# A delta-rule attention with two expert layers: the queries' transposes, a down step and the split of the next weights put elsewhere

## The chip, the core and the metric

One NeuronCore of a Trainium2 chip runs the whole kernel in one launch. The metric is device microseconds from start to end of an execution; less is better. The engines are PE (TensorE, the matrix products), DVE (VectorE), ACT (ScalarE), POOL (GpSimd) and SP (SyncE, which here only issues transfers). Each has its own list of instructions, done in order, and waits for the others by semaphores.

## The reference

Three stages follow one another. Only what the change touches is shown in full.

```python
# 1: delta rule, batch 4, 8 heads, 768 tokens, head width 48
k_n = k / (norm(k) + 1e-06)
for t in range(S):
    y[:, :, t] = einsum('bhd,bhde->bhe', q[:, :, t], state)
    v_old = einsum('bhde,bhd->bhe', state, kt)
    state = state + bt * einsum('bhd,bhe->bhde', kt, vt - v_old)
# 2: four experts, N = 3072 tokens, D = 384, F = 1024
out += p[:, e:e + 1] * (maximum(x @ w1[e], 0.0) @ w2[e])
# 3: gated layer, F = 1536
(sigmoid(x @ w_gate) * (x @ w_val)) @ w_out
```

## The kernel before, in words

**Attention.** The 768 tokens are cut into 6 chunks of 128, and the 32 heads into two groups of 16. A window `w` (12 of them) is one chunk of one group. Within a window the recurrence becomes a triangular system of 128 by 128 per head. Its inverse is built by doubling: levels `l0` to `l4` work on blocks of 32 (line 790), each for two halves of 8 heads; a level's product goes from PE to DVE (mask, then a 32 by 32 transpose, lines 641 and 643) and to ACT (copy, line 561), and the next level needs both. The steps `m32y`, `m32z`, `m64y`, `m64z` then put blocks together.

The order of the work is written out by hand, in `slot(w, p, lev, rec, pre, moe)`. All engines run through the same list of calls, and each engine's own functions `lev`, `rec`, `pre`, `moe` say what it does at a call. A slot mixes four kinds of work: the levels of window `w`; the recurrence of window `w - 1` (`r(...)`: `u0` line 848, `au_a` and `au_b` lines 854 and 857, `u2` line 865, `y` lines 872 and 876, `s` line 884, whose sum into the state is DVE line 687); the preparation of window `w + 1` (`n(...)`); and a part of the first expert for window `w - 2` (`up` line 947, `down` line 956). In the first two slots, where there is no such window, PE does four stand-in products on constants (line 935) in the place of each up or down.

Preparation: `turn` transposes the unit keys on PE (line 892) and ACT copies them out; `product` is keys times keys (line 900), which DVE masks into `A` and `Ah` (lines 728 and 732); `first` (POOL line 528, DVE line 721) makes from `Ah` what level `l0` of the next slot needs. `turn_q` transposes the queries: 4 transposes for each half of the heads on PE, into `bank[0]` and `bank[1]`, and one ACT copy of 128x512 each into `KQ`. `product_q` is keys times queries (line 900 too), which DVE masks into `QK`, two operations of 128x512 for each half (line 739). `product_q` of half 1 writes the same two banks as half 0 and so waits until DVE has emptied them.

With window 1's second `turn_q`, DVE also normalizes the experts' weights (`early.normalize`, lines 999 to 1005).

**Experts.** The other half of expert 0 and the experts 1 to 3 run over 6 chunks of 512 tokens. For each block of 128 hidden units `f` PE does `up` (9 matmuls of 128x512), ACT makes the rounded high part (line 1130), DVE the low part (line 1165), and PE does `down` (12 matmuls of 128x384) one `f` later (lines 1194 to 1196). The weights of the next expert come by DMA as soon as the raw buffers are free and are split by ACT (`split1` line 1113 and `split2` line 1120) and by POOL (line 1100). Expert 0 has only 4 blocks `f` left, so ACT splits two blocks of each weight after each `f` there.

**Gated layer.** It is not touched.

The change lies in `slot`, in `run` and in the ACT block of `experts`, whose `split2` holds ACT until the raw weights have landed:

```python
def split2(e, f):
    if e:
        act.wait_ge(w2_in, 16 * e)
```

Of the kernel before, what the change touches and what calls it, by code (L numbers as in the profile page):

```python
# [60 lines left out]
def past(eng, semaphore, count):  # L61

    if not isinstance(count, int) or count > 0:
        eng.wait_ge(semaphore, count)


def delta_rule_attention(nc, q, k, v, beta, consts, places, x_hi, x_lo, ident, id_in, early, room, x_first, x_first_in):
# [9 lines left out]
    with ctx:  # L77
# [126 lines left out]
        def slot(w, p, lev, rec, pre, moe):  # L204

            m, has_next = w - 2, w < NW - 1

            def r(step, o):
                if w > 0 and not (step == "s" and w == NW - 1):
                    rec(step, w - 1, 1 - p, o)  # L210

            def n(step, which=None):
                if has_next:
                    pre(step, w + 1, 1 - p, which)

            def both(step):
                for hf in range(2):
                    lev(step, w, p, hf)

            def down(window, t, *fs):  # L220
                for f in fs:
                    moe("down", window, t, f)

            def up(f):
                for part in range(2):
                    moe("up", m, f, part)

            pre("value", w, p, None)
            both("l0")
            r("u0", 0)  # L230
            moe("weigh", m - 1, 0)
            n("square")
            down(m - 1, 1, 0, 1)
            both("l1")
            r("u0", 1)
            down(m - 1, 1, 2, 3)
            both("l2")
            moe("weigh", m - 1, 1)
            n("norm")
            n("unit", 0)  # L240
            n("unit", 1)
            r("au_a", 0)
            up(0)
            moe("low", m, 0)
            both("l3")
            r("au_b", 0)
            up(1)
            moe("low", m, 1)
            both("l4")
            both("blocks")  # L250
            both("quads")
            r("au_a", 1)
            n("turn", 0)
            rec("z", w, p, 0)
            both("m32y")
            r("au_b", 1)
            up(2)
            moe("low", m, 2)
            n("turn", 1)
            r("u2", 0)  # L260
            rec("z", w, p, 1)
            up(3)
            moe("low", m, 3)
            r("u2", 1)
            both("m32z")
            n("product", 0)
            r("y", 0)
            both("m64y")
            n("product", 1)
            down(m, 0, 0, 1)  # L270
            both("m64z")
            r("y", 1)
            pre("product_q", w, p, 0)
            r("s", 0)
            pre("product_q", w, p, 1)
            down(m, 0, 2, 3)
            r("s", 1)
            n("first", 0)
            n("first", 1)
            n("turn_q", 0)  # L280
            n("turn_q", 1)

        def run(lev, rec, pre, moe):
            for step, which in (("square", None), ("norm", None), ("unit", 0), ("unit", 1),
                                ("turn", 0), ("turn", 1), ("product", 0), ("product", 1),
                                ("first", 0), ("first", 1), ("turn_q", 0), ("turn_q", 1)):
                pre(step, 0, 0, which)
            for w in range(NW):
                slot(w, w % 2, lev, rec, pre, moe)
            m = NW - 2  # L290
            moe("weigh", m - 1, 0)
            for o in range(2):
                rec("u0", NW - 1, 1, o)
                for f in range(2 * o, 2 * o + 2):
                    moe("down", m - 1, 1, f)
            moe("weigh", m - 1, 1)
            for o in range(2):
                rec("au_a", NW - 1, 1, o)
                moe("up", m, o, 0)
                rec("au_b", NW - 1, 1, o)  # L300
                moe("up", m, o, 1)
                moe("low", m, o)
            rec("u2", NW - 1, 1, 0)
            moe("up", m, 2, 0)
            rec("u2", NW - 1, 1, 1)
            for o in range(2):
                rec("y", NW - 1, 1, o)
            moe("up", m, 2, 1)
            moe("low", m, 2)
            for part in range(2):  # L310
                moe("up", m, 3, part)
            moe("low", m, 3)
            for t in range(2):
                for f in range(KH):
                    moe("down", m, t, f)
                moe("weigh", m, t)
            for f in range(KH):
                for part in range(2):
                    moe("up", NW - 1, f, part)
                moe("low", NW - 1, f)  # L320
            for t in range(2):
                for f in range(KH):
                    moe("down", NW - 1, t, f)
                moe("weigh", NW - 1, t)
# [31 lines left out]
        with nc.Block() as block:  # L356
# [106 lines left out]
            def _(pool):  # L463
# [85 lines left out]
                def none(*_):  # L549
                    return  # L550

                run(lev, rec, pre, none)

            @block.scalar
            def _(act):
# [69 lines left out]
                def moe(step, m, f, part=1):  # L625
                    if step == "up" and part == 1 and m >= 0:
                        act.wait_ge(up_rdy, KH * m + f + 1)
                        past(act, dn_rdy, 2 * m)
                        nc.scalar.activation(hs[0][:, f, :], ebank[f % 2][:, 0:2 * P], ACT.Relu).then_inc(hh_done, 1)

                run(lev, rec, pre, moe)

            @block.vector
            def _(dve):
# [120 lines left out]

                nc.vector.memset(XTf[:, :, :].bitcast(F32), 0.0).then_inc(x_zeroed, 1)
                run(lev, rec, pre, moe)

            @block.tensor
# [250 lines left out]
def experts(nc, x_hi, x_lo, w1, w2, early, acc, w1raw, w2raw, w1_in, x_first, x_first_in, ahead):  # L1010
# [4 lines left out]
    E, D, F = w1.shape  # L1015
    N = x_hi.shape[1]
    KD, KF, NCK = D // P, F // P, N // T
    ctx = ExitStack()
    with ctx:
# [14 lines left out]
        def steps(g, e):  # L1034
            return KH * g if e == 0 else KF * g - (KF - KH) * NCK

        def todo(e):
            return KH if e == 0 else KF
# [17 lines left out]
        with nc.Block() as block:  # L1056
# [47 lines left out]
            @block.scalar  # L1104
            def _(act):
                def split1(e, f):

                    if e:
                        act.wait_ge(w1_in, 16 * e)
                    else:  # L1110
                        act.wait_ge(early.raw_in, 64)
                    raw, cols = w1raw if e else early.raw1, slice(P * f, P * (f + 1))
                    nc.scalar.activation(w1s[e % 2][0][:, :, cols], raw[:, :, cols], ACT.Copy).then_inc(w1_hi, 1)  # L1113
# [5 lines that stand above are left out]
                    raw = w2raw if e else early.raw2  # L1119
                    nc.scalar.activation(w2s[e % 2][0][:, f, :], raw[:, f, :], ACT.Copy).then_inc(w2_hi, 1)  # L1120

                def chunk(g, e, splits=None):
                    at = steps(g, e)
                    for f in range(todo(e)):
                        if isinstance(g, int) and g == 0 and f:
                            split2(0, f - 1)
                        i = f % NHB
                        act.wait_ge(h_rdy, at + f + 1)
                        past(act, o_used, at + f + 1 - NHB)
                        nc.scalar.activation(hs[i][0][:, :], bank[i][:, :], ACT.Relu).then_inc(hh_done, 1)  # L1130
                        if splits is not None:
                            per = KF // todo(e)
                            for n in range(per * f, per * (f + 1)):
                                split1(splits, n)
                                split2(splits, n)
                    if isinstance(g, int) and g == 0:
                        split2(0, KH - 1)

                for f in range(KH):
                    split1(0, f)  # L1140
                for e in range(E):
                    chunk(NCK * e, e)
                    chunk(NCK * e + 1, e, e + 1 if e + 1 < E else None)
                    with act.Fori(NCK * e + 2, NCK * (e + 1)) as g:
                        chunk(g, e)

            @block.vector
# [401 lines left out]
```

## Time and profile before

| | us |
|---|---|
| median of 3 runs | 1708.73 |
| lowest and highest | 1707.78, 1711.89 |
| profiled execution | 1704.52 |
| its span, first to last instruction | 1702.7 |
| PE busy | 1632.3 (96%) |
| DVE busy | 654.5 (38%) |
| ACT busy | 436.1 (26%) |
| POOL busy | 279.3 (16%) |

The attention with its part of expert 0 takes the first 520 us, the experts go to about 1235 us, the gated layer to the end. A slot of the attention takes about 38 us. PE is busy in nearly all of the span; what is left over is in short waits. The mean granted TensorE clock over the span is 0.987 of full speed: 1 is 2.4 GHz and 0.5 is 1.2 GHz, the only two levels in this trace.

### The profile page before, as it was taken

What the parts mean: (1) busy time and instruction counts of PE and PEld (TensorE: products, weight loads), DVE (VectorE), ACT (ScalarE), POOL (GpSimd) and SP (SyncE); (2) the same over time, 40 slices, a digit from 0 to 9 for tenths busy, and PEclk for the clock granted to TensorE, in tenths of its full rate; (3) what the DMA queues carried; (4) which work ended last, traced back from release to release, by engine and by line L of the source; (5) the groups of instructions that cost most, each with busy time, mean ns of one, the idle gap of its engine ahead of it and who ended that gap; (6) DMA issues with size and microseconds to landing.
All of it is one profiled execution on the core that took longest, in us unless ns stands there. A gap on an engine that the chain in (4) does not pass through costs nothing. (4 is left out here: it accounts for less than half of the span.)

```text
span 1702.7 us, 35068 instructions
## 1 busy us (share of the span) xinstructions
PE 1632.3 (96%) x14630; PEld 1462.4 (86%) x14630; DVE 654.5 (38%) x1193; ACT 436.1 (26%) x852; POOL 279.3 (16%) x404
## 2 busy tenths in 40 slices
PE   5899999999988999999999999999989999999999
PEld 4788888888877899999999999999878888888887
DVE  5777777777632232222222222222243222222221
ACT  3333334444312212211121111111143222222222
POOL 4654444444300300300003000000000000000000
PEclk9999999999999999999999999999999999999999
DMA  6335433344137241111212112211030000000000
GB/s 136 66 89 136 98 96 91 89 99 98 49 110 279 86 156 66 38 64 48 111 37 75 37 37 67 73 38 37 0 112 29 19 19 1 19 0 18 0 19 19
DMA packets 171731, 113.23 MB, mean 66 GB/s; under 512 B 82224, under 2 KB 151216, under 8 KB 171600
## 3 DMA queue, kind: packets, MB, share of 16 engines
q1 hardware_dynamic: 171600, 111.33, 22.2%
q8 instruction: 101, 1.65, 0.4%
q14 instruction: 30, 0.25, 0.0%
HBM read 92.43 MB, written 18.87 MB: 65 GB/s over the span
## 5 line engine op out<-in xcount | busy, mean ns | idle before, releaser
L1165 DVE SCALAR_TENSOR_TENSOR hl<-ebank,hh 128x512 fp32r<-128x512 f32 x168 | 116.4, 693 | 503.8 <-ACT hh L1130 503.8
L1130 ACT ACTIVATE hh<-ebank 128x512 fp32r<-128x512 f32 x168 | 100.6, 599 | 577.9 <-PE ebank L1196 577.9
L1194 PE MATMUL ebank<-w2l,hh 128*128 128x384 f32 x672 | 226.4, 337 | 3.8 <-DVE hl L1165 3.8
L1196 PE MATMUL ebank<-w2h,hh 128*128 128x384 f32 x672 | 226.6, 337 | 0.0
L1195 PE MATMUL ebank<-w2h,hl 128*128 128x384 f32 x672 | 225.9, 336 | 0.0
L1194 PEld LDWEIGHTS ebank<-w2l,hh 128*128 128x128 f32 x672 | 126.4, 188 | 10.7 <-DVE hl L1165 4.2
L1195 PEld LDWEIGHTS ebank<-w2h,hl 128*128 128x128 f32 x672 | 126.3, 188 | 6.0
L1390 DVE TENSOR_TENSOR prod<-gbank,gate 128x512 f32<-128x512 f32 x72 | 49.7, 690 | 209.6 <-ACT gate L1337 209.6
L1196 PEld LDWEIGHTS ebank<-w2h,hh 128*128 128x128 f32 x672 | 126.3, 188 | 0.0
L1315 POOL COPY stage<-acc 128x1536 f32 (+1 forms) x5 | 7.4, 1475 | 601.5 <-POOLq L1056 323.6
L1194 PE MATMUL ebank<-room,w1h 128*128 128x512 f32 x252 | 99.3, 394 | 4.3 <-DVE w1l L1152 4.3
L1196 PE MATMUL ebank<-room,w1h 128*128 128x512 f32 x252 | 100.4, 399 | 0.0
L1195 PE MATMUL ebank<-room,w1l 128*128 128x512 f32 x252 | 100.3, 398 | 0.0
L1196 PE MATMUL ebank<-xh,w1h 128*128 128x512 f32 x252 | 99.7, 396 | 0.0
L1195 PE MATMUL ebank<-xh,w1l 128*128 128x512 f32 x252 | 99.6, 395 | 0.0
L1424 PE MATMUL gbank<-wol,mh 128*128 128x384 f32 x288 | 98.4, 342 | 0.7 <-DVE ml L1394 0.7
L1194 PE MATMUL ebank<-xl,w1h 128*128 128x512 f32 x252 | 98.4, 391 | 0.0
L1426 PE MATMUL gbank<-woh,mh 128*128 128x384 f32 x288 | 97.1, 337 | 0.0
L1425 PE MATMUL gbank<-woh,ml 128*128 128x384 f32 x288 | 96.8, 336 | 0.0
L1337 ACT ACTIVATE gate<-gbank 128x512 f32<-128x512 f32 x72 | 43.0, 598 | 208.9 <-PE gbank L1426 208.9
L1100 POOL TENSOR_TENSOR w1l<-w1raw,w1h 128x1024 fp32r<-128x1024 f32 x9 | 21.4, 2410 | 381.7 <-ACT w1h L1113 381.7
L528 POOL TENSOR_TENSOR XY<-Ah,c 32x256 f16<-32x256 f16 x96 | 73.0, 761 | 47.4 <-DVE Ah L732 39.1
(175 smaller groups left out, 3313.4 us busy)
## 6 DMA issues: line engine op xcount, KB each, us to landing
room<-x_hi SPq DMA_DIRECT2D x12, 768.0 KB, 4.2
room<-x_lo SPq DMA_DIRECT2D x12, 768.0 KB, 5.7
xh<-x_hi SPq DMA_DIRECT2D x12, 768.0 KB, 4.2
xl<-x_lo SPq DMA_DIRECT2D x12, 768.0 KB, 5.8
brep<-in_beta SPq DMA_DIRECT2D x24, 256.0 KB, 5.7
k_raw<-in_k SPq DMA_DIRECT2D x12, 384.0 KB, 4.0
v_raw<-in_v SPq DMA_DIRECT2D x12, 384.0 KB, 5.7
q<-in_q SPq DMA_DIRECT2D x12, 384.0 KB, 6.2
```

The costliest lines, as they stand in the source:

```text
L528: last = nc.gpsimd.tensor_tensor(XY[which][quarter(b), :, 0, :], Ah[p][quarter(b), half(which), quarter(b)], mask, ALU.mult)
L1100: last = nc.gpsimd.tensor_tensor(parts[1][:, t, :], raw[:, t, :], parts[0][:, t, :].bitcast(F32), ALU.subtract)
L1130: nc.scalar.activation(hs[i][0][:, :], bank[i][:, :], ACT.Relu).then_inc(hh_done, 1)
L1165: nc.vector.scalar_tensor_tensor(out=hs[i][1][:, :], in0=bank[i][:, :], scalar=0.0, in1=hs[i][0][:, :].bitcast(F32), op0=ALU.max, op1=ALU. ...
L1194: mm(dst, stat[0], mov[1], start=first, stop=False)
L1195: mm(dst, stat[1], mov[0], start=False, stop=False)
L1196: return mm(dst, stat[0], mov[0], start=False, stop=last)
L1337: nc.scalar.activation(gate[:, :], bank[f % 2][:, :], ACT.Sigmoid).then_inc(gate_done, 1)
L1390: nc.vector.tensor_tensor(prod[:, :], bank[2 + f % 2][:, :], gate[:, :], ALU.mult)\
L1424: mm(dst, stat[0], mov[1], start=first, stop=False)
L1425: mm(dst, stat[1], mov[0], start=False, stop=False)
L1426: return mm(dst, stat[0], mov[0], start=False, stop=last)
```

## The change

Three things are put elsewhere; nothing is added or left out.

1. `turn_q` of a window stood at the end of the slot before it, after `first`, for both halves. Now it stands in the window's own slot: half 0 between levels `l2` and `l3` (before `up(0)`), half 1 between `l3` and `l4` (before `up(1)`). Window 0's goes from the steps ahead of the first slot to its slot, and `early.normalize` goes with window 1's.
2. `down(m, 0, 2, 3)` stood after the second `product_q`; now it stands between the two.
3. In the experts, ACT splits expert 1's weights during chunk 2 of expert 0 instead of chunk 1. Experts 2 and 3 are split in chunk 1 as before.

```diff
             r("au_a", 0)
+            pre("turn_q", w, p, 0)
             up(0)
             moe("low", m, 0)
             both("l3")
             r("au_b", 0)
+            pre("turn_q", w, p, 1)
             up(1)
...
             pre("product_q", w, p, 0)
             r("s", 0)
+            down(m, 0, 2, 3)
             pre("product_q", w, p, 1)
-            down(m, 0, 2, 3)
             r("s", 1)
             n("first", 0)
             n("first", 1)
-            n("turn_q", 0)
-            n("turn_q", 1)
...
                                 ("turn", 0), ("turn", 1), ("product", 0), ("product", 1),
-                                ("first", 0), ("first", 1), ("turn_q", 0), ("turn_q", 1)):
+                                ("first", 0), ("first", 1)):
...
-                    chunk(NCK * e, e)
-                    chunk(NCK * e + 1, e, e + 1 if e + 1 < E else None)
-                    with act.Fori(NCK * e + 2, NCK * (e + 1)) as g:
+                    turn = 2 if e == 0 else 1
+                    for c in range(turn):
+                        chunk(NCK * e + c, e)
+                    chunk(NCK * e + turn, e, e + 1 if e + 1 < E else None)
+                    with act.Fori(NCK * e + turn + 1, NCK * (e + 1)) as g:
                         chunk(g, e)
```

PE at the end of slot 1, where the stand-in L935 is in the place of the down step. L900 are the two `product_q`, L884 the two `s`, L892 the queries' transposes, and L790 is level `l0` of the next slot.

```order
 L900 MATMUL bank<-KQ,kT 128x128 x8
 L884 MATMUL bank<-Uu,kn_0 64x48 x8
+L935 MATMUL bank<-c 128x256 x8
 L900 MATMUL bank<-KQ,kT 128x128 x8
-L935 MATMUL bank<-c 128x256 x8
 L884 MATMUL bank<-Uu,kn_0 64x48 x8
-L892 MATMUL bank<-ident,q_0 128x128 x8
 L790 MATMUL bank<-Ah,Yn 32x32 x64
 L848 MATMUL bank<-room 128x48 x8
```

The down step has moved up by one product, and between the last `s` and `l0` nothing is left.

PE in slot 2, from level `l2` (first row) to the first matmuls of `up(0)` (L947); L854 is `au_a`.

```order
 L790 MATMUL bank<-XY,Yn 32x64 x64
 L854 MATMUL bank<-U_0,A_1 128x48 x4
+L892 MATMUL bank<-ident,q_0 128x128 x4
 L947 MATMUL bank<-xs_l,w1half_h 128x256
 L947 MATMUL bank<-xs_h,w1half_l 128x256
```

Four transposes now stand between `au_a` and `up(0)`; the other four stand in the same way between `au_b` and `up(1)`.

ACT in the experts. First before, from the last block of chunk 0 (first row) into chunk 1:

```order
L1130 ACTIVATE hh<-ebank 128x512
L1120 ACTIVATE w2h<-w1raw 128x384
L1130 ACTIVATE hh<-ebank 128x512
L1113 ACTIVATE w1h<-w1raw 128x3x128
L1120 ACTIVATE w2h<-w2raw 128x384
L1113 ACTIVATE w1h<-w1raw 128x3x128
L1120 ACTIVATE w2h<-w2raw 128x384
L1130 ACTIVATE hh<-ebank 128x512
```

Then the changed kernel, from the same place:

```order
L1130 ACTIVATE hh<-ebank 128x512
L1120 ACTIVATE w2h<-w1raw 128x384
L1130 ACTIVATE hh<-ebank 128x512 x5
L1113 ACTIVATE w1h<-w1raw 128x3x128
L1120 ACTIVATE w2h<-w2raw 128x384
```

The split of `w1raw` and `w2raw` stood behind the first block of chunk 1 and now stands behind the first block of chunk 2.

## Rows read from the trace of the kernel before

**Rows 1.** Stretches: start:end, us, busy of PE, PEld, DVE, ACT, POOL, clock, DMA

```profile
253.49:291.35 37.86, 36.26 (x733) 32.78 (x733) 29.22 (x63) 15.52 (x36) 17.62 (x29) 1.00 0.42 100
172.04:212.11 40.07, 37.62 (x732) 33.94 (x733) 29.25 (x63) 15.59 (x36) 17.62 (x29) 0.96 0.41 96
212.11:253.49 41.38, 39.13 (x732) 35.45 (x733) 29.32 (x63) 15.64 (x36) 17.61 (x29) 0.92 0.38 91
443.74:495.00 51.26, 47.21 (x766) 44.02 (x767) 23.71 (x50) 14.70 (x34) 10.35 (x20) 0.93 0.21 60
```

**Rows 2.** Waits of PE in slots 1 to 11: us, times, longest

```profile
PE bank L900 <- DVE QK L739: 10.8, 11, 1.5
PE bank L790 <- DVE Yn L721: 3.6, 10, 0.4
PE bank L790 <- ACT XY L561: 1.4, 3, 0.7
PE bank L790 <- DVE Yn L643: 0.9, 4, 0.3
```

**Rows 3.** Timeline of PE at the end of slot 9

```profile
399.10 0.67 PE L884 MATMUL bank<-Uu,kn 128*64 128x48 f32 x16
400.70 1.16 PE L900 MATMUL bank<-KQ,kT 64*128 64x128 f32 x16 [0.92 <-DVE QK L739]
401.79 0.44 PE L956 MATMUL bank<-w2half_l,hs_h 128*128 128x384 f32 x1
403.03 0.67 PE L884 MATMUL bank<-Uu,kn 128*64 128x48 f32 x16
403.63 1.09 PE L892 MATMUL bank<-ident,q 128*128 128x128 f32 x8
405.09 0.70 PE L790 MATMUL bank<-Ah,Yn 32*32 32x32 f16 x64 [0.36 <-DVE Yn L721]
```

**Rows 4.** Timeline of DVE there

```profile
401.90 1.29 DVE L739 TENSOR_TENSOR QK<-bank,c 128x512 f32<-128x512 f32 x2 [0.64 <-PE bank L900]
403.75 0.72 DVE L687 TENSOR_TENSOR S<-S,bank 64x192 f32<-64x192 f32 x2 [0.56 <-PE bank L884]
404.50 0.77 DVE L721 STREAM_TRANSPOSE Yn<-XY 128x256 f16<-128x256 f16 x2
```

**Rows 5.** Timeline of PE: four transposes of keys and what follows

```profile
380.45 0.62 PE L892 MATMUL bank<-ident,kn 128*128 128x128 f32 x4
380.90 1.03 PE L831 MATMUL bank<-S,KQ 128*128 128x96 f32 x8
```

**Rows 6.** Experts: chunks 1 and 2 of expert 0

```profile
545.35:567.74 22.39, 18.58 (x86) 16.46 (x85) 4.96 (x8) 8.99 (x21) 4.44 (x2) 0.92 0.63 235
567.74:584.41 16.67, 16.67 (x86) 15.14 (x85) 4.96 (x8) 2.39 (x4) 10.48 (x10) 1.00 0.28 95
```

**Rows 7.** Timelines of ACT and PE in chunk 1

```profile
552.65 0.52 ACT L1120 ACTIVATE w2h<-w2raw 128x384 fp32r<-128x384 f32 x1 [4.79 <-DMA w2raw<-in_moe_w]
555.36 0.45 PE L1194 MATMUL ebank<-w2l,hh 128*128 128x384 f32 x1 [3.81 <-DVE hl L1165]
```

**Rows 8.** The transfer of chunk 2's x_lo: issue, then us to landing; and its first use

```profile
543.95 1.49 SPq L1066 DMA_DIRECT2D room<-x_lo  x1
...
room<-x_lo SPq DMA_DIRECT2D x1, 768.0 KB, 12.4
...
565.37 0.39 PE L1194 MATMUL ebank<-room,w1h 128*128 128x512 f32 x1
```

**Rows 9.** Timeline of PE: idle time that no other engine explains

```profile
176.46 0.29 PE L790 MATMUL bank<-XY,Yn 32*32 32x64 f16 x15 [0.98 <-issue]
217.06 0.74 PE L848 MATMUL bank<-room 128*128 128x48 f32 x5 [0.74 <-issue]
142.41 0.28 PE L947 MATMUL bank<-xs_h,w1half_l 128*128 128x256 f32 x1 [1.45 <-issue]
```

**Rows 10.** The stretch of half clock after the second of these

```profile
219.00:225.50 6.50, 6.50 (x150) 6.09 (x149) 4.29 (x14) 1.91 (x5) 2.26 (x3) 0.50 0.01 3
```

## The prediction

> **What bounds the kernel now.** I read the stretches by slot first [rows 1]: an undisturbed slot of the attention takes 37.86 us, and PE is busy for 36.26 of them, so work that is added to PE's stream lengthens the slot unless it falls into a wait. Next I read the list of PE's waits over slots 1 to 11 [rows 2]. Two come in every slot: for DVE's `QK` (10.8 us in 11) and for DVE's `Yn` ahead of level `l0` (3.6 us in 10). The timelines of PE and DVE at the end of slot 9 show where they lie [rows 3, 4]. Then the stretches of the experts [rows 6], the waits of ACT and PE in chunk 1 [rows 7], the transfers beside them [rows 8], and last the granted clock, which is below 1 in two of the three slots shown, and what PE did before it fell [rows 1, 9, 10]. The reader should see that the change touches three separate places, two in the slot and one in the experts.
>
> **The experts' split.** In chunk 1 ACT sits idle 4.79 us until `w2raw` has landed [rows 7]. Behind it in ACT's list stands the high part of the next block, so DVE's low part comes late and PE sits idle 3.81 us. Chunk 1 takes 22.39 us at a mean clock of 0.92, the next one, with nothing to split, 16.67 [rows 6]. Moved to chunk 2, the split finds both weights landed. Its copies, 8.99 - 2.39 = 6.6 us of ACT's time [rows 6], lie beside 16.67 us of products on PE. Three more chunks of 16.67 us stand between chunk 2 and the first use of the split weights, so nothing comes late there. Gain: 22.39 - 16.67 = 5.7 us. What is late next would be chunk 2's `x_lo`: issued at 543.95, landed 12.4 later at 556.35; its chunk starts at 565.37 now and would start at 559.7 [rows 8], so 3.3 us are in hand. Bounds: 5.7 and, if only PE's wait went, 3.8.
>
> **Down between the two products.** Now `s` of half 0 starts at 399.10 and holds PE for 0.60 (403.63 - 403.03 for its twin), so the down step would start at 399.70 and, 1.24 long (403.03 - 401.79), end at 400.94 [rows 3]. The banks are free at about 400.70, where the second `product_q` starts now. So the whole wait of 0.92 is covered and the product starts 0.24 later than now.
>
> **The slot's end.** Now 405.09 - 400.70 = 4.39 us pass from the second product to `l0` [rows 3]. On DVE [rows 4] the `QK` operations start 1.20 after the product does (401.90), take 1.29, then DVE idles 0.56 for `s`, adds the state (from 403.75), transposes from 404.50, and `l0` starts 0.59 later. In the changed order `s` follows the product at once, at 400.94 + 1.09 = 402.03, and is ready before DVE wants it, so the 0.56 goes: QK from 402.14 to 403.43, state from 403.43, `Yn` from 404.18, `l0` at 404.77. That is 0.32 us earlier per slot, 10 slots with a next level and a full end: -3.2. DVE's own chain now holds `l0`, and PE has nothing for the time from 402.63 to 404.77: a wait of 2.1 us where the transposes of queries and 0.36 us of waiting stood. The order shown ahead confirms that `l0` follows `s` directly. After slot 11 there is no `l0`, so the 0.92 is gained whole: -0.9.
>
> **The queries' transposes in the levels.** Four transposes hold PE for 0.45 us (380.90 - 380.45) [rows 5], so two sets add 0.9 to a stretch in which PE shows hardly a wait: 12 x 0.9 = +10.8. They cover the wait for `Yn` at `l4` (0.9 in 4 slots [rows 2]): -0.9. The ACT copies come with them, two of 128x512, in front of the high part and of `l4`'s copy. ACT is busy 15.5 of 37.9 us [rows 1], and no PE step waits for it in these slots except the 1.4 us below, so I cost them at nothing; if they delayed `l4` by their own length it would be the worst bound, which I put at one transposing step, 0.45 a slot, +5. Could the 0.9 a slot be hidden altogether? Only if the levels were held by their own chain PE-DVE-ACT; the bound below is then 0 instead of +10.8. I take +10.8, since the fill between levels leaves PE no idle time in the row list but these.
>
> **Slot 1.** The normalization leaves DVE's list ahead of `l0`'s mask. PE's three waits for ACT's `XY`, 1.4 us [rows 2], come mostly from it: I take -1.0 (bounds 0 and -1.4). In its new place between `l3` and `l4` I cost it at nothing; bound +1.
>
> Without the clock: -5.7 - 3.2 - 0.9 + 10.8 - 0.9 - 1.0 = -0.9 us.
>
> **The clock.** The trace of before shows what a short idle can do in this part of a slot. At 176.46 PE had sat idle 0.98, at 217.06 0.74 [rows 9], both among the short products of the levels and `u0`. After each, the granted clock fell to 1.2 GHz; after the second it stayed there for the whole 6.5 us shown [rows 10]. The slot of the first takes 40.07 us, that of the second 41.38 [rows 1]. Less the undisturbed 37.86 and the idle itself, a fall costs 40.07 - 37.86 - 0.98 = 1.2 us or 41.38 - 37.86 - 0.74 = 2.8 us. The new wait of 2.1 us stands between `s` and `l0`, in the same thin stretch, and every one of the 11 ends of slots has it. On the other side, 1.45 us of idle amid the dense `up` steps (142.41) [rows 9], and the 0.92 before the product, cost no fall. Bounds: no fall, 0; the long one each time, 11 x 2.8 = +31. I take the mean of the two, 2.0, at 10 of 11 ends, +20.0, less what the falls of before in slots 4, 5 and 11 cost and would no longer add (1.2 + 2.8 + 2.8 = 6.8, the third taken like the second by its mean clock, 0.93): +13.2.
>
> The Trainium skill, "TensorE: Matmul & The Clock Gate", has two rules for this. Its section "HAM oscillation — how this bites in real kernels" counts only idle stretches longer than these; by it nothing is added, which is the second rival below. Its section "A second HAM failure mode: psum-queue depth-cycling" says that frequent short idles between groups of matmuls are enough to make the clock swing. The trace agrees with the second for 0.98 and 0.74 us.
>
> **Sum.** 1704.5 - 0.9 + 13.2 = 1716.8 by the profiled execution. The median of before is 4.2 above that execution; its idle times and falls differ from run to run, and some of these can't come twice, so I carry half of it: 1719.
>
> **Rivals.**
> - The long fall at every end of a slot: 1704.5 - 0.9 + 30.8 - 6.8 = 1727.6, with the half 1730. For it: two of the three falls I priced were long. Chance 0.1.
> - The clock holds through 2.1 us, or falls only in the slots where it did: 1704.5 - 0.9 = 1703.6, and 1707.8 by the median. For it: no fall follows the waits of 0.92 and 0.36, 21 of them, nor the 1.45. Against it: those have dense work around them. Chance 0.15.
> - Falls at about half the ends, 5 more us or so: 1704.5 - 0.9 + 10 - 6.8 = 1706.8, by the median up to 1711. Chance 0.1.
> - The other side: the levels have slack that the list of waits hides. The transposes then fill it and only the gains stay: 1704.5 - 5.7 - 3.2 - 0.9 - 0.9 - 1.0 = 1692.8, by the median 1697. It decides from the point where each of the two sets costs under 0.1 us in place of 0.45, and needs a steady clock. For it: four `l4` waits show the chain close behind PE. Against it: the other levels show none. Chance 0.15.
> - The split of the weights gains nothing, because `x_lo` or the sums of chunk 0 hold chunk 2 up: +5.7 on any of these. 3.3 us in hand speak against it; 0.03, inside the others.
>
> **How the numbers follow.** The forecast, falls at most ends of slots, has 0.5 and reaches by itself from 1712 to 1727. A measurement of this kernel can't tell less than 0.3% (5.1 us, so 1703.6 to 1713.9) from no change. Faster: the fourth case and a little of the second, 0.17. Within: most of the second and third and the low edge of the forecast, 0.25. Slower: the rest, 0.58. The range of 8 in 10 goes from 1700 to 1728: it takes in the second and third case and leaves out most of the fourth and the top of the first.
>
> **What would show it.** In the new profile PE's wait for `QK` should be near 1 us in all (it was 10.8); its wait for `Yn` of line 721 should be near 11 x 2 = 22 us (it was 3.6); the clock by slot should be about 0.92 to 0.96 nearly everywhere; chunk 1 of the experts should take 16.7 us. The prediction is wrong if the slots are at a clock of 1.00 and at or below 38.4 us, or if `l0` waits clearly less than 1.5 us.

## The result, and the profile after

The changed kernel takes 1727.05 us (median of 4 runs, 1725.82 to 1728.37), the kernel before 1710.31 beside it. The ratio on record is 1.0117, with a 95% interval of 1.0067 to 1.0168 (the two medians alone give 1.0098). It is slower, on the side that was forecast and inside the range by 1 us, but by 16.7 us where 8.7 to 10.3 followed from the forecast of 1719. The ratios here and below leave out runs more than 1.5% above the fastest of the same kernel (at most 7 of 29, of the kernel before), the medians don't, so the two can differ by some tenths of a per cent. The mean granted clock is 0.966 or 0.967 in the four runs. The profiled execution took 1726.90, its span is 1725.1.

The head of the page of the changed kernel: busy us (share of the span) x instructions, then the clock in 40 slices.

```profile
span 1725.1 us, 35061 instructions
PE 1656.6 (96%) x14630; PEld 1486.8 (86%) x14630; DVE 656.1 (38%) x1193; ACT 436.8 (25%) x852; POOL 278.7 (16%) x404
PEclk9898999899888999999999999999999999999999
```

PE has the same 14630 matmuls and is busy for 24.3 us more. It doesn't do more, it does it more slowly: the clock is below full in the slices of the attention.

The waits of PE from 50 to 520 us, which answer to [rows 2]:

```profile
PE bank L790 <- DVE Yn L721: 21.6, 11, 2.0
PE bank L900 <- DVE QK L739: 1.1, 2, 0.8
```

The wait for `QK` is gone (10.8 to 1.1 us), and the wait for `Yn` ahead of `l0` has grown from 3.6 to 21.6. The end of slot 9 on PE, and then on DVE, against [rows 3] and [rows 4]:

```profile
417.22 0.44 PE L956 MATMUL bank<-w2half_l,hs_h 128*128 128x384 f32 x1
...
418.48 1.16 PE L900 MATMUL bank<-KQ,kT 64*128 64x128 f32 x16
419.57 0.67 PE L884 MATMUL bank<-Uu,kn 128*64 128x48 f32 x16
422.22 0.70 PE L790 MATMUL bank<-Ah,Yn 32*32 32x32 f16 x64 [1.98 <-DVE Yn L721]
```

```profile
419.68 1.29 DVE L739 TENSOR_TENSOR QK<-bank,c 128x512 f32<-128x512 f32 x2 [0.90 <-PE bank L900]
420.89 0.71 DVE L687 TENSOR_TENSOR S<-S,bank 64x192 f32<-64x192 f32 x2
421.63 0.77 DVE L721 STREAM_TRANSPOSE Yn<-XY 128x256 f16<-128x256 f16 x2
```

DVE's `QK`, state and `Yn` now stand one behind the other without a gap, and they alone hold `l0`. From the second product to `l0` it is 3.74 us (forecast 3.83, before 4.39).

The stretches by slot (start:end, us, busy of the five, clock, DMA share, GB/s), against [rows 1]: three of the ten slots 1 to 10, one of them the only one without a fall, and slot 11 with what follows it.

```profile
137.40:179.51 42.11, 40.07 (x732) 36.53 (x733) 29.32 (x63) 15.82 (x35) 17.63 (x29) 0.88 0.50 128
343.57:384.25 40.68, 38.61 (x732) 35.08 (x733) 29.20 (x63) 15.55 (x35) 17.64 (x29) 0.92 0.40 93
384.25:422.22 37.97, 35.81 (x732) 32.64 (x733) 29.23 (x63) 15.51 (x35) 17.61 (x29) 1.00 0.44 102
463.06:516.00 52.94, 49.94 (x738) 46.39 (x739) 22.04 (x47) 15.19 (x34) 10.34 (x20) 0.81 0.21 60
```

At full clock a slot takes 37.97 us, 0.11 more than before. In all others of these ten the clock is below 1 (0.84 to 0.96). Pieces of three of the low stretches:

```profile
56.30:69.60 13.30, 13.30 (x210) 10.72 (x214) 6.39 (x18) 5.42 (x11) 3.51 (x4) 0.50 0.01 3
138.20:148.00 9.80, 9.80 (x157) 8.74 (x157) 4.74 (x11) 3.68 (x7) 2.00 (x2) 0.50 0.74 240
346.30:352.90 6.60, 6.60 (x146) 5.56 (x144) 3.06 (x7) 2.32 (x5) 1.91 (x2) 0.50 0.09 26
```

Each begins within 3 us behind a start of `l0` (55.16, 137.40, 343.57). The slots 1 to 11 hold 10 such stretches around `l0`, 85 us together; nine begin up to 2.8 us behind a start of `l0`, one (260.77) in the idle just ahead of it. Before there were 4 in these slots, 20 us, none of them so close behind `l0`. These 65 us are most of the 68 us that the whole trace has more at half clock; another stretch of 13.7 us follows at 509.95, behind an idle of 2.08 us that no engine explains. In such a stretch PE shows no idle time and takes about twice as long for the same matmuls: eight of `u0` (line 848) are 1.87 us at 138.17 against 1.04 at 385.04.

```profile
138.17 1.87 PE L848 MATMUL bank<-room 128*128 128x48 f32 x8
...
385.04 1.04 PE L848 MATMUL bank<-room 128*128 128x48 f32 x8
```

Slot 0, before and then changed. The 33.0 us of before hold 3.4 us at half clock (from 37.84); the changed kernel's 31.5 hold none.

```profile
23.92:56.91 32.99, 25.27 (x592) 20.28 (x593) 23.00 (x49) 12.20 (x27) 18.95 (x32) 0.95 0.30 67
23.62:55.16 31.54, 24.22 (x593) 19.47 (x594) 22.18 (x47) 11.93 (x27) 18.31 (x32) 1.00 0.31 72
```

Chunk 1 of the experts, against [rows 6]: 16.68 us where it was 22.39, with ACT's split copies gone from it.

```profile
574.05:590.73 16.68, 16.68 (x85) 15.15 (x84) 4.96 (x8) 2.40 (x4) 0.00 (x0) 1.00 0.86 316
```

### The profile page after: what moved, and what is told of

The parts are those of the page before. It is cut to its first block and busy times, and to the rows that moved or that the text cites. A ratio compares the mean times of both kernels' runs of the same rounds, so it can differ in the third digit from the quotient of the medians.

```text
span 1725.1 us, 35061 instructions
## 1 busy us (share of the span) xinstructions
PE 1656.6 (96%) x14630; PEld 1486.8 (86%) x14630; DVE 656.1 (38%) x1193; ACT 436.8 (25%) x852; POOL 278.7 (16%) x404
## 5 line engine op out<-in xcount | busy, mean ns | idle before, releaser
L561 ACT ACTIVATE XY<-bank 128x256 f16<-128x256 f32 (+1 forms) x120 | 55.2, 470 | 163.1 <-DVE Yt L641 162.5
```

Of the source, the lines that this page charges most:

```text
L561: return nc.scalar.activation(dst, src, ACT.Copy, scale=scale)
```

## The experiments

The mean clock of a run tells how long PE was at half clock: 2 x (1 - clock) x span, since the levels are 1 and 0.5 (the clock of a run is on record to 0.001, which is 3.4 us of that). That makes every run a measurement of two things. The kernel before spreads widely over its runs, 1693 to 1729 us in 29 of them, and a line through these is 1685.4 + 0.446 x (us at half clock). So nearly all of its spread is the clock. The table has the medians, the 95% interval of the ratio to the kernel before in the same session, and the mean us at half clock over the runs. (Two of the ten runs with 5 products, 4222 and 6239 us, were disturbed; they stand in its median, which is 1718.08 without them, and don't count in the ratio and the half clock.)

| kernel | median us | before beside it | ratio | half clock, us | before's |
|---|---|---|---|---|---|
| changed | 1727.05 | 1710.31 | 1.0067 to 1.0168 | 115 | not taken |
| split only | 1706.57 | 1709.25 | 0.9949 to 1.0025 | 50 | 55 |
| down only | 1711.93 | 1709.25 | 1.0015 to 1.0077 | 71 | 55 |
| queries only | 1729.75 | 1709.25 | 1.0093 to 1.0206 | 110 | 55 |
| changed, 5 products in the gap | 1719.29 | 1706.03 | 1.0028 to 1.0109 | 84 | 47 |
| changed, 12 products | 1706.38 | 1709.25 | 0.9980 to 1.0048 | 61 | 55 |
| changed, 16 products | 1687.79 | 1706.03 | 0.9871 to 0.9937 | 18 | 47 |
| the same, split early | 1689.82 | 1703.88 | 0.9892 to 0.9944 | 17 | 42 |
| split and down | 1708.70 | 1706.03 | 0.9983 to 1.0055 | 70 | 47 |
| split and down, 7 products | 1698.94 | 1706.03 | 0.9928 to 0.9995 | 45 | 47 |
| before, idle filled | 1704.71 | 1703.88 | 0.9972 to 1.0022 | 40 | 42 |
| before, levels thickened | 1714.41 | 1706.85 | 0.9997 to 1.0057 | 48 | 49 |
| before, both | 1695.40 | 1706.85 | 0.9910 to 0.9961 | 19 | 49 |

**Theory and rivals.** Theory A: the loss is the granted clock, which falls because PE stands idle about 2 us ahead of `l0`, in a stretch with only short products. Rival D: the loss is the transposes among the levels. Others are in the expectations.

**The three parts alone.** The split only:

```diff
-                    chunk(NCK * e, e)
-                    chunk(NCK * e + 1, e, e + 1 if e + 1 < E else None)
-                    with act.Fori(NCK * e + 2, NCK * (e + 1)) as g:
+                    turn = 2 if e == 0 else 1
+                    for c in range(turn):
+                        chunk(NCK * e + c, e)
+                    chunk(NCK * e + turn, e, e + 1 if e + 1 < E else None)
+                    with act.Fori(NCK * e + turn + 1, NCK * (e + 1)) as g:
```

> The kernel before with only the split of expert 1's weights a chunk later. Theory A (the 16.7 us lost come from the clock, which falls at the idle ahead of level l0) says nothing against this edit: chunk 1 goes from 22.4 to 16.7 us and the kernel gains 5 to 6 us, near 1704.5 against 1710.3. Rival B (chunk 1's wait only goes over to chunk 2, or the gain is eaten up): within 2 us of the kernel before.

Its chunk 1 takes 16.68 us as it should, but the whole is only 2.7 us faster, and the interval holds no change: against a spread of 30 us this run can't tell the expected 5 to 6 us from rival B's 2.

Down only:

```diff
             r("s", 0)
+            down(m, 0, 2, 3)
             pre("product_q", w, p, 1)
-            down(m, 0, 2, 3)
```

> The kernel before with only the down step between the two products with queries. PE's wait for QK should go from 0.92 to about 0 a slot, l0 should come 0.3 us earlier, and its wait for Yn should grow from 0.36 to about 1.1 us, behind the queries' transposes. Theory A: this idle is about half of the changed kernel's 1.98 and dense work (the transposes) lies ahead of it, so the clock falls seldom: 0 to 3 falls more, the time between 4 us less and 5 us more than before. Rival C (any idle over about 1 us ahead of l0 brings the fall): 8 or more falls, 10 to 25 us more.

A calm slot at full clock becomes shorter, 37.50 us from 37.86. The first row is such a slot; the other three are the end of one on PE:

```profile
332.64:370.14 37.50, 36.18 (x733) 32.76 (x733) 29.12 (x63) 15.52 (x36) 17.57 (x29) 1.00 0.43 101
```

```profile
367.48 0.67 PE L884 MATMUL bank<-Uu,kn 128*64 128x48 f32 x16
369.04 1.06 PE L892 MATMUL bank<-ident,q 128*128 128x128 f32 x8 [0.88 <-DVE QK L739]
370.14 0.69 PE L790 MATMUL bank<-Ah,Yn 32*32 32x32 f16 x64
```

I had the idle in the wrong place: the queries' transposes write the banks that DVE still empties, so they wait for `QK` and `l0` doesn't wait at all. The wait has moved by one product, from dense neighbours to behind `s`. Over the runs 16 us more are spent at half clock (71 against 55). By the ratio the kernel comes out 0.15 to 0.77% slower, by the medians 2.7 us, although its calm slots are faster. In the profiled execution the slots 1 to 11 hold four stretches at half clock, as before, but 36 us of them where there were 20. That is what theory A allowed in number, and at the upper end or above in time; rival C (8 or more falls, 10 us more at least) has the falls against it.

Queries only (transposes among the levels, down step and split as before), against the kernel before:

```diff
             r("au_a", 0)
+            pre("turn_q", w, p, 0)
...
             r("au_b", 0)
+            pre("turn_q", w, p, 1)
...
-            n("turn_q", 0)
-            n("turn_q", 1)
```

> The kernel before with only the queries' transposes among the levels. The wait for QK stays 0.92, the wait for Yn ahead of l0 becomes about 1.2 to 1.4 us with only the short products of s ahead of it. Theory A: the clock falls at most ends of slots, slots of 40 us and more, 15 to 28 us over the kernel before. Rival D (the transposes lengthen the levels by their own 0.9 us and the clock counts for little): a slot at full clock of 38.8 us, 5 to 11 us over the kernel before.

It is as slow as the whole change, 20 us over the kernel before, where theory A had 15 to 28. Two of its waits and two of its slots:

```profile
PE bank L790 <- DVE Yn L721: 14.7, 11, 1.4
PE bank L900 <- DVE QK L739: 11.0, 11, 1.8
```

```profile
180.78:222.23 41.45, 38.74 (x733) 34.99 (x734) 29.32 (x63) 15.62 (x35) 17.63 (x29) 0.92 0.40 93
222.23:266.31 44.08, 41.69 (x732) 37.96 (x733) 29.38 (x63) 15.85 (x35) 17.63 (x29) 0.85 0.37 86
```

In this profile the clock falls in every one of the slots 1 to 11, within 3 us behind `l0`; the idle ahead of it is 1.39 us (0.85 ahead of slot 1). The profiled execution, 1747.90, is the slowest of its six. None of the slots 1 to 10 takes rival D's 38.8 us at full clock; they take 40.2 to 44.2. So the queries' part carries the loss.

**Filling the gap of the changed kernel.** These tell theory A from rival D: the work on PE grows, the idle goes. The products write a bank that nothing reads and are not used.

```diff
             n("first", 1)
+            moe("fill", m, 0)
...
+                    if step == "fill":
+                        pe.wait_ge(consts_in, 32)
+                        for _ in range(12):
+                            mm(ebank[1][:, 0:2 * P], eye, small_eye, start=True, stop=True)
```

With 12, 5 and 16 of them:

> The changed kernel with 12 more products of constants (128x256 each, about 1.5 us together, into a bank that nothing reads) on PE between the last s and level l0. They compute nothing that is used. Theory A: they fill the idle, the clock stays at 2.4 GHz, the slots go back to about 38.0 us and the kernel gets 25 us faster than the changed one: about 1700. Rival D (the loss is PE work among the levels): more work on PE gains nothing, 1727 or more.

> The changed kernel with 5 more products of constants (0.6 us, not used by anything) between the last s and level l0; the idle ahead of l0 should be 1.4 us. Theory A (the fall follows from how little PE does in the stretch around l0): between the changed kernel (1727, 115 us at half clock over the run) and the one with 12 (1706.4, 61 us): about 1715 to 1724, 80 to 105 us at half clock. Rival E (any filler ends the effect): 1706.

> The changed kernel with 16 such products (2.0 us), which fill the idle whole. Theory A: fewer falls than with 12: 1695 to 1704, 25 to 50 us at half clock. Rival F (12 had already done what filling can do, the rest of the falls comes from elsewhere in the levels or from instruction fetch): as with 12, 1703 to 1710.

0, 5, 12, 16 products: 1727, 1719, 1706, 1688 us. More work on PE takes 39 us away. With 12 the kernel stayed 6 us above the 1700 I expected, with 5 it was as expected, and with 16 the kernel came out faster and calmer than expected (18 us at half clock, not 25 to 50). With 5 the idle is 1.33 us and falls stay; with 12 it is 0.57 and a slot is either calm or not:

```profile
207.21:245.21 38.00, 37.22 (x744) 33.76 (x745) 29.19 (x63) 15.45 (x35) 17.58 (x29) 1.00 0.42 100
245.21:285.90 40.69, 40.04 (x745) 36.27 (x746) 29.23 (x63) 15.63 (x35) 17.56 (x29) 0.92 0.40 93
```

With 16 an idle of 0.13 us is left. The head of that page, and two slots:

```profile
span 1686.5 us, 35445 instructions
PE 1638.0 (97%) x14822; PEld 1469.7 (87%) x14822; DVE 654.0 (39%) x1193; ACT 434.4 (26%) x852; POOL 279.1 (17%) x404
PEclk9999999999999999999999999999999999999999
```

```profile
168.32:206.29 37.97, 37.67 (x748) 34.13 (x749) 29.22 (x63) 15.51 (x35) 17.56 (x29) 1.00 0.42 99
206.29:244.26 37.97, 37.66 (x748) 34.13 (x749) 29.24 (x63) 15.48 (x35) 17.57 (x29) 1.00 0.41 100
```

192 matmuls more and 18.6 us less of PE busy time than the changed kernel. In the slots 0 to 11 the clock didn't fall at all; the first fall is at 495 us, in the tail of the attention. The ten runs lie within 1685.99 to 1689.57. It is about 1% faster than the kernel before and the fastest of all that were run. Theory A is shown in this: what PE does in the 2 us ahead of `l0` decides over the falls, and rivals D, E and F fall. Whether it is the idle as such or the lack of dense work there is not separated, since the products end both.

**The split with a quiet clock.** The same with 16 products, but with the split in chunk 1 again:

```diff
-                    turn = 2 if e == 0 else 1
-                    for c in range(turn):
-                        chunk(NCK * e + c, e)
-                    chunk(NCK * e + turn, e, e + 1 if e + 1 < E else None)
...
+                    chunk(NCK * e, e)
+                    chunk(NCK * e + 1, e, e + 1 if e + 1 < E else None)
```

> The changed kernel with 16 products of constants ahead of l0, but with expert 1's weights split in chunk 1 as before. With the clock quiet this prices the later split: 1693.5 (5.7 more than 1687.8) if the edit is worth what chunk 1 shows; within 1 us of 1687.8 if its gain is given back elsewhere.

The later split is worth about 2.0 us here (1689.82 - 1687.79, over two sessions; by the two ratios, 0.9918 and 0.9904, 2.4), not 5.7. Chunk 1 and PE's wait in it:

```profile
532.35:551.61 19.26, 17.04 (x86) 15.13 (x85) 4.96 (x8) 8.99 (x21) 4.44 (x2) 1.00 0.73 273
```

```profile
PE ebank L1199 <- DVE hl L1170: 2.2, 1, 2.2
```

In this run `w2raw` landed 9.7 us after its issue, not 11.3 as in the profile of before; PE waited 2.2 us instead of 3.81, and no fall followed. So 3.1 of the 5.7 us of [rows 6] (22.39 - 19.26) were that run's landing time and a fall.

**What would keep the kernel before calm.** Split and down, without and with 7 products between `s` and the transposes at the slot's end:

```diff
             r("s", 1)
+            moe("fill", m, 0)
             n("first", 0)
```

> The same without the filler. Both gains at full clock (about 4 and 4 us) but an idle of 0.9 us ahead of the queries' transposes. Theory A: the falls of the kernel with the down step alone (71 us at half clock) stay: 1702 to 1710. Rival: the two gains simply add to the kernel before: 1700 to 1702.

> The kernel before with the split of the weights a chunk later, the down step between the two products with queries, and 7 products of constants (0.87 us, not used by anything) between the last s and the queries' transposes, which stay at the slot's end. Theory A: no idle is left there, a slot at full clock takes 37.5 us, and falls are rarer than in the kernel before: 1690 to 1700, faster than both kernels. Rival: the filler costs its own time or brings nothing: 1700 to 1708.

Without them the two gains are eaten by 22 us more at half clock; theory A. With them it is 0.05 to 0.72% faster than the kernel before. The half clock goes back to that of the kernel before (45 against 47) but not lower, so my expectation of rarer falls than before was wrong. Dense work at the slot's end alone does not calm this order below that. The next three runs ask why: the kernel before with 7 and 4 products in its two idle places, with 4 products at each of the two places among the levels, and with both. (Those among the levels write the banks of the queries and first wait until these are free.)

```diff
+            moe("fill", m, 7)
             pre("product_q", w, p, 1)
...
             n("turn_q", 1)
+            moe("fill", m, 4)
...
             r("au_a", 0)
+            pre("thick", w, p, 0)
             up(0)
...
             r("au_b", 0)
+            pre("thick", w, p, 1)
             up(1)
```

> The kernel before, with products of constants that nothing uses in its two idle places: 7 (0.87 us) ahead of the second product with queries, 4 (0.5 us) between the queries' transposes and level l0. Theory A: its own falls come from the same thin stretch, so they go too: 1688 to 1695, 20 to 30 us at half clock over the run instead of some 50. Rival G (the kernel before has its falls from instruction fetch among the levels, and filling changes nothing): 1703 to 1710.

> The kernel before with 4 products of constants (0.5 us, not used by anything) at each of the two places among the levels at which the changed kernel has its transposes; those stay at the slot's end. Theory H (the falls of the kernel before start in the thin stretch of the levels, so dense work there stops them): slots at full clock of 38.6 to 38.8 us, but 20 to 30 us at half clock instead of 42 to 55: the time within 4 us of the kernel before on either side. Rival I (the two idles at the slot's end bring the falls): 40 us or more at half clock and 5 to 12 us slower.

> The same, and the two idle places at the slot's end filled as well (7 and 4 products). Theory H: it is as calm as the changed kernel with 16 (18 us at half clock), so 1686.5 - 47 x 0 + 0.9 x 12: about 1695 to 1700, a spread of runs of under 5 us. Rival J (it was the exact order of the changed kernel that kept the clock, not dense work in both places): 35 us or more at half clock, 1703 to 1712, spread as before.

Neither alone does anything to the half clock (40 against 42, 48 against 49). Both together bring it to 19 against 49, and the kernel, with over 200 products that nobody uses, is faster than before by 0.4 to 0.9%. So for the first of the three my theory was wrong (it expected 20 to 30 us at half clock), and for the second H was; rival G and rival I each came true in the time. For the third H came true in time and half clock (its spread is 6.7 us, not under 5), and rival J falls. What holds is that in this order the falls go only when a dense piece stands in both places at once. Where the idle at the slot's end is filled, a fall is still seen after an idle that no engine explains, among the levels (PE, slot 9 of that kernel):

```profile
361.29 0.54 PE L792 MATMUL bank<-XY,Yn 32*32 32x64 f16 x47
362.52 0.30 PE L792 MATMUL bank<-XY,Yn 32*32 32x64 f16 x17 [0.70 <-issue]
...
364.07 0.34 PE L962 MATMUL bank<-w2half_h,hs_l 128*128 128x384 f32 x1
364.24 0.38 PE L962 MATMUL bank<-w2half_h,hs_h 128*128 128x384 f32 x1
364.42 0.52 PE L962 MATMUL bank<-w2half_l,hs_h 128*128 128x384 f32 x1
```

Matmuls of one shape, for which 0.34 us is the time at full clock, go to 0.52. With both places thick (slots 6 and 7 of the last kernel) the slots stay at full clock:

```profile
247.79:286.22 38.43, 38.04 (x753) 34.32 (x753) 29.32 (x63) 15.64 (x36) 17.57 (x29) 1.00 0.43 99
286.22:324.55 38.33, 38.09 (x752) 34.33 (x752) 29.32 (x63) 15.63 (x36) 17.55 (x29) 1.00 0.42 98
```

This fits the changed kernel too: its transposes among the levels are such dense work, and there products in one place were enough (17 us at half clock with 16, where the order of before with its end filled kept 40). How the work among the levels does it stays open. The idle that no engine explains is itself rarer with it: in the slots 1 to 10 of the profiled executions it comes to 4.1, 3.4, 3.0, 2.8, 4.2 and 2.1 us in the kernels without anything at these places, and to 0.4, 0.9, 0.7, 2.4, 0.5 and 0 in those with the queries' transposes there. With the 4 products there it was 6.6 us, and 1.3 when the slot's end was filled as well. One execution each can't say which part of the calm is fewer such idles and which is that the clock holds through them, and no run shows what causes them.

## Why the prediction had direction and mechanism right and the size wrong

- **Down between the products, and DVE's chain at the slot's end: right.** `QK`'s wait went from 10.8 to 1.1 us, `Yn`'s to 21.6 (forecast about 22), `l0` follows the product after 3.74 us (3.83).
- **The clock at the ends of slots: the step that failed, right in mechanism and number, too small in price.** 10 falls in the slots 1 to 11 were forecast and 10 came. I priced one at 2.0 us, the mean of a short and a long one of before (1.2 and 2.8). The nine falling slots among 1 to 10 take 41.10 us in the mean against 37.97 for the calm one: 3.1 each, above even the long one. The error is in the length of a stretch: those two lasted 3.4 and 6.8 us, the ten last 8.5 in the mean (85 / 10). Per us at half clock the price is about the same, 1.2 / 3.4 = 0.35 and 2.8 / 6.8 = 0.41 before, 3.1 / 8.0 = 0.39 here (the nine). I took falls that follow a chance idle among the levels as models for one that comes ahead of them. Why these last longer is not shown; my reading is that they begin before the whole row of short products. Over the whole run it is 115 us at half clock against 55 (29 runs of before). With before's 0.446 for both that is 60 x 0.446 = 26.7 us; but for the changed kernel the runs with 16 and with no product give (1727.1 - 1687.6) / (115 - 18) = 0.407, and then it is 0.407 x 115 - 0.446 x 55 = 22.3. Either is far above the 13.2 of the sum.
- **The rival that came true.** The first one, the long fall at every end, had 1727.6 for the profiled execution, which took 1726.9. I gave it 0.1, and the range left out most of it, so that the range holds 1727.05 is in part luck. So is the closeness of 1727.6: its falls were priced at 2.8, not 3.1, and at 11 ends, not 10, and it had the rest too slow.
- **Everything but the clock: -5 to -9 us, forecast -0.9.** It is what is left of 1727.1 - 1709.8 = 17.3 (the means) with either price of the clock: 17.3 - 22.3 = -5.0, or 17.3 - 26.7 = -9.4. The first is the better one, since its price comes from the changed order itself, whose slot at full clock is 37.97 us with the 16 products as without. A set of four transposes costs 0.38 us, not 0.45 (391.65 to 392.03), and the waits at `l4` went in all slots. A slot at full clock is 0.11 us longer, where the terms came to 0.5: that is some 4 us. In slot 0, `l0` to `l0`, the 1.45 us from 32.99 to 31.54 are the 3.4 us at half clock that before had there (3.4 x 0.446 = 1.5), so without the clock nothing changed, where I had costed 0.9. Against these stands the split, which brought 3.7 less than forecast. What remains, 3 us or more, was not assigned by an experiment; the idle that no engine explains, 4.1 us in the slots 1 to 10 of before and 0.4 in the changed kernel, is of that size.
- **The experts' split: right in the wait, too large as a price.** It is worth 2.0 us with a quiet clock.
- **The two misses had opposite signs.** The clock's term was short by 9 to 13.5 us, the others too high by 4 to 8.5; the forecast is only 8 us off because they partly cancel. The median's offset to the profiled execution, half of which I carried, was the clock's spread too. And the kernel before is noisier than the 0.3% that I took from three runs: 36 us lie between the lowest and the highest of 29.
- **The rival by the Trainium skill.** By the section "HAM oscillation — how this bites in real kernels" of "TensorE: Matmul & The Clock Gate" only longer idles count; the traces contradict it, with falls after 1.98 us (changed), 1.39 (queries only) and 0.57 (12 products). The section "A second HAM failure mode: psum-queue depth-cycling" of that page says that frequent short idles between groups of matmuls are enough; the trace agrees, with 10 falls for 11 idles of 1.83 to 1.98 us.

## What to carry to other kernels

A wait that is taken away comes back behind the next chain; ask what PE does around the place where it comes back. Where all neighbours are short products, an idle of one or two microseconds can cost more by the clock than its own length, here 3 us. When a PE-bound kernel spreads over runs, put its times against the mean granted clock first: here a line of 0.446 us per us at half clock explained the spread of the kernel before (its slope was 0.41 for the changed one, so it doesn't carry over exactly), and 16 unused products a slot in the gap were worth more than any of the three edits.

## What the runs showed that I had not expected

- The kernel before loses about 19 to 24 us to the clock on its own (42 to 55 us at half clock, by the line), and filling one thin place of two changed nothing of it (40 and 48), while filling both left 19.
- The spread over runs goes with it: 1693 to 1729 for the kernel before, 1686.0 to 1689.6 with 16 products.
- A transfer of 1.5 MB behind another landed 9.7 us after its issue in one run (16 products, split early) and 11.3 in another (the kernel before), with the same program in that part.
